# The last token group of a fused RWKV, MLP and soft-MoE kernel worked in two halves, the first one gathered behind step 92

## The reference

```python
# recurrence, per batch and head (4 x 8 x 768 x 48)
cur = einsum('bhd,bhe->bhde', u[None] * kt, vt)
y[:, :, t] = einsum('bhd,bhde->bhe', rt, state + cur)
state = wt[:, :, :, None] * state + einsum('bhd,bhe->bhde', kt, vt)
# dense MLP
h = x @ w_in                                   # 3072x384 @ 384x2048
g = h * clip(h + 3.0, 0.0, 6.0) / 6.0
x2 = g @ w_out
# soft mixture
logits = x2 @ phi                              # 3072 x 32
d = exp(logits - logits.max(0)); d /= d.sum(0) + 1e-09
slot_input = (d.T @ x2).reshape(8, 4, 384)
slot_out[e] = maximum(slot_input[e] @ w1[e], 0.0) @ w2[e]
c = exp(logits - logits.max(1)); c /= c.sum(1) + 1e-09
out = c @ slot_out
```

## Time and profile before

| quantity | us |
| --- | --- |
| median of 3 runs | 408.07 |
| lowest and highest | 407.99, 408.35 |
| the profiled execution | 409.01 |
| its span in the profile | 406.3 |
| TensorE busy in the span | 391.6 |
| VectorE, ScalarE, GpSimd busy | 329.2, 208.1, 210.5 |

### The profile page before, as it was taken

The page is one execution under the profiler, slowest core; times in us unless marked ns, Lnnn a source line. Parts: engine busy times, 40 slices in busy tenths (PEclk is TensorE's granted clock), DMA queues, the critical chain, the costliest instruction groups (busy, mean ns, idle before and its releaser), DMA issues.

```text
span 406.3 us, 10112 instructions
## 1 busy us (share of the span) xinstructions
PE 391.6 (96%) x3977; PEld 210.1 (52%) x3977; DVE 329.2 (81%) x536; ACT 208.1 (51%) x449; POOL 210.5 (52%) x200
## 2 busy tenths in 40 slices
...
GB/s 236 338 407 328 137 67 63 126 235 294 39 128 106 27 124 128 113 20 126 128 115 15 128 114 63 81 128 60 2 2 311 54 423 377 224 298 412 388 112 356
DMA packets 16543, 69.37 MB, mean 171 GB/s; under 512 B 2160, under 2 KB 3184, under 8 KB 14832
## 3 DMA queue, kind: packets, MB, share of 16 engines
...
...
## 4 chain that ended last, share of the span: by engine, by line
PE 74%; DVE 10%; issue 6%; ACT 5%; DMA 2%; POOL 0%; SPq 0%; DVEq 0%; POOLq 0%; ACTq 0%
PE hid L617 13%; PE hid L619 12%; PE hid L618 12%; PE l_ps L665 5%; PE sc_ps L501 4%; PE l_ps L728 3%; PE hid L887 3%; PE inc_ps L530 2%; PE y_ps L600 2%; DVE gated L1076 1%; ACT relu L1495 1%; PE hid L868 1%; PE k_ps L511 1%; PE sc_ps L868 1%; PE y_ps L576 1%
## 5 line engine op out<-in xcount | busy, mean ns | idle before, releaser
L617 PE MATMUL hid<-x_split,w_split 128*128 128x512 f16 x285 | 108.3, 380 | 0.3 <-DVE gated L1076 0.3
L619 PE MATMUL hid<-x_split,w_split 128*128 128x512 f16 x285 | 108.0, 379 | 0.0
L618 PE MATMUL hid<-x_split,w_split 128*128 128x512 f16 x285 | 108.0, 379 | 0.0
L1495 ACT ACTIVATE relu<-hid,three 128x512 f32<-128x512 f32 x95 | 65.1, 685 | 82.2 <-PE hid L619 81.7
L1076 DVE SCALAR_TENSOR_TENSOR gated<-relu,hid 128x512 f32<-128x512 f32 x95 | 64.4, 678 | 24.3 <-ACT relu L1495 23.9
L1097 DVE STREAM_TRANSPOSE ring<-gated 128x512 f32<-128x512 f32 x96 | 68.2, 711 | 3.2
L1701 POOL TENSOR_TENSOR att<-att 128x1024 f16<-128x1024 f32 x20 | 40.2, 2011 | 39.7 <-ACT att L1383 39.7
L617 PEld LDWEIGHTS hid<-x_split,w_split 128*128 128x128 f16 x285 | 27.7, 97 | 36.7 <-issue 6.3
L619 PEld LDWEIGHTS hid<-x_split,w_split 128*128 128x128 f16 x285 | 27.8, 98 | 33.7
L1710 POOL TENSOR_TENSOR att<-att 112x512 f32<-112x512 f32 x21 | 25.5, 1215 | 36.5 <-DVE att L976 26.9
L618 PEld LDWEIGHTS hid<-x_split,w_split 128*128 128x128 f16 x285 | 27.8, 98 | 24.7
...
## 6 DMA issues: line engine op xcount, KB each, us to landing
...
att<-w_dram SPq DMA_DIRECT2D x3, 1536.0 KB, 9.6
...
stage<-w_in_dram SPq DMA_DIRECT2D x2, 1536.0 KB, 13.9
...
```

The source lines that it names most:

```text
L617: pe.matmul(hid[s % 2][:], high, x_high, start=(q == 0), stop=False)
L618: pe.matmul(hid[s % 2][:], high, x_low, start=False, stop=False)
L619: last = pe.matmul(hid[s % 2][:], low, x_high, start=False, stop=(q == KT - 1))
L1495: nc.scalar.activation(relu_tile(s), hid[s % 2][:], ACT.Relu, bias=three[:], scale=GATE / H_SCALE)\
```

## The change

The last group (LAST = 80 = its first step) is worked in two halves of tokens throughout. Steps 80 to 87 make all 16 tiles for the first 256 tokens, two tiles in a step, steps 88 to 95 those for the second. Each step has 18 products of 128 x 256 in place of nine of 128 x 512. The logits are added two steps (four products) at a time, behind the steps listed in `LAST_LOGITS`. The first half's logits are copied, folded, lowered, exponentiated, transposed and summed at steps 89 to 91, and its gather (32 products 32 x 512) stands on TensorE behind step 92 (`gather_half(0, r)`). ScalarE copies the four banks of sums to `dg_half` at steps 93 and 94. Behind step 95 the second half does the same with its own maximum and a second scale `late_alpha`, and its gather of 32 products goes to four other banks (`late_dg_bank`). The fold takes three parts: `acc`, `dg_half` and `dg_last`. The inverse sum is applied later, as the scale of ScalarE's `slot_part` copy.

```diff
+LAST = STEPS - FT
+HALF_STEPS = FT // 2
+GH = GT // 2
-        c_bank = [hid[1], hid[0], sc_bank[1]]
+        late_dg_bank = [y_ps[:, :], inc_ps[:, :], hid[0][:, :], hid[1][:, :]]
+        fold_bank = sc_bank
+        c_bank = [sc_bank[0], hid[0], sc_bank[1]]
+        LAST_LOGITS = {4: 0, 5: 1, 7: 2, 8: 3, 10: 4, 12: 5, 14: 6}
...
+            def half_tile(to, i, half):
+                tokens = (EARLIER, LATER)[half]
+                for q in range(KT):
+                    high, low = w16[:, i, 0, q, :], w16[:, i, 1, q, :]
+                    x_high, x_low = (x16[:, (C - 1) % 2, a, q, tokens] for a in range(2))
+                    pe.matmul(to, high, x_high, start=(q == 0), stop=False, skip_group_check=True)
+                    pe.matmul(to, high, x_low, start=False, stop=False, skip_group_check=True)
+                    last = pe.matmul(to, low, x_high, start=False, stop=(q == KT - 1), skip_group_check=True)
+                return last
...
+                if s >= LAST:
+                    half, pair = divmod(i, HALF_STEPS)
+                    for t in range(2):
+                        last = half_tile(hid[s % 2][:, t * GH:(t + 1) * GH], 2 * pair + t, half)
...
+            def gather_half(half, r):
+                if r == 0:
+                    pe.wait_ge(gated_turned, LAST + HALF_STEPS * (half + 1))
+                    pe.wait_ge(weight_turned, C + half)
+                    pe.wait_ge(acc_added, 4 * (C - 1))
+                    if half:
+                        pe.wait_ge(logits_done, C)
+                        pe.wait_ge(cT_done, 1)
+                for a in range(4):
+                    for c in range(4):
...
+                if s >= LAST and i in LAST_LOGITS:
+                    add_last_logits(LAST_LOGITS[i], range(4))
+                if s == LAST + HALF_STEPS + 1:
                     fold_last_logits(0)
+                if s == STEPS - 4:
+                    for r in range(2):
+                        gather_half(0, r)
...
+            add_last_logits(7, (0, 1))
+            add_last_logits(7, (2, 3))
+            last_natural_logits(0)
+            fold_last_logits(1)
+            last_natural_logits(1)
+            turn_c(1)
+            stay_warm(2, k_ps)
+            for r in range(2):
+                gather_half(1, r)
             for half in range(2):
                 for a in range(4):
                     fold_earlier(a, half)
+                for a in range(4):
+                    fold_first_half(a, half)
                 for a in range(4):
                     fold_last(a, half)
-            stay_warm(1, y_ps)
+            stay_warm(1, k_ps)
             for half in range(2):
                 apply_w_out(half)
-            stay_warm(2, y_ps)
+            turn_c(0, 0, 5)
...
+            half_maximum(1)
+            copy_cT(1)
+            turn_half_weight(1)
+            sum_half_weight(1)
...
+            def weigh_half(half):
+                g, tokens = C - 1 + half, (EARLIER, LATER)[half]
+                act.wait_ge(neg_max_done, g + 1)
+                act.wait_ge(run_sum_done, C - 1)
+                nc.scalar.activation(weight[:, tokens], last_l[half], ACT.Exp, bias=run_neg[g % 2]).then_inc(weight_done, 1)
...
+                if s in (STEPS - 3, STEPS - 2):
+                    first = 2 * (s - STEPS + 3)
+                    for a in range(first, first + 2):
+                        act.wait_ge(dg_ready, 16 * C)
+                        nc.scalar.activation(dg_half[a], dg_bank[a], ACT.Copy).then_inc(dg_half_copied, 1)
```

344 lines of the change are left out of this document (179 added, 165 removed).

## The result

The changed kernel takes **411.97 us** (median, 411.55 to 413.23), the kernel before 408.21 beside it: a ratio of 1.0093, interval 1.0069 to 1.0117. It is slower by 3.8 us; 411.1 was forecast, with 409.7 to 412.6 around it. The sign and the mechanism came out as predicted. But that the stages which the prediction prices add up to +3.1 for +3.0 is in part luck, since its terms missed by 0.7 us in each direction, and another 1.0 us was lost in a place that it did not look at.

The account below looks back on a forecast made before the run. TensorE was taken to bound the steps and the gather onward, with a latency chain between. Terms 4.42 - 0.24 - 2.15 + 1.05 - 0.05 gave +3.0 us on the median of 408.07: 411.1 us, range 409.7 to 412.6.

Parts of the forecast that it names:

- The third rival: Steps 86 to 95 move at the pace of relu and gate, so insertions cost nothing; 407.1 us, chance 0.05.
- The clock, the fourth: Behind step 95 the emptier tail lets TensorE's clock fall, slowing gather and folds; 414 to 416 us, chance 0.05.
- 1, products of 256 columns: In nine steps, 18 products replace nine and add 0.03 us a step; +0.27 us.
- 2, logits: In the steps, five insertions of four products at 0.65 replace two of eight at 1.10; +1.05 us.
- 3, the fold: Between steps 89 and 90, the first half's logits are folded; +0.6 us, bounds 0.5 and 0.75.
- 4, the first gather: Behind step 92, 32 products, half a whole gather, plus switching once more; +2.35 us, bounds 2.2 and 2.6.
- 5, the softmax ahead of the gates: First half's maximum, exponential and sums delay gates 90 and 91, mostly covered by logits; +0.15 us, bounds 0 and 1.2.
- 6, ScalarE's copies: Copies of the first sums behind the relu of steps 93 and 94; no cost, without cover at most 0.5 us.
- 7 and 8, from step 95 to the gather, and the gather: Fewer logit passes but a tile copy before the second gather, -0.24 us; 32 gather products for 64, -2.15 us.
- 9, the folds: Behind the second gather, 24 fold products replace 16 at 0.13 us each; +1.05 us, lower bound 0.
- 10, the projection to the experts: Five transposes replace two unread products, and small softmax instructions just fit beside; -0.05 us, upper bound +0.5.
- 11, loads: The loads of w2 for the experts land early enough that nothing waits for them; 0 us.

Follow-up runs that it names:

- e3: The changed kernel with the first half's gather done twice behind step 92, the second over the first; 413.14 us, ratio 1.0123 to the kernel before.
- e1: The changed kernel with the first half's gather moved from behind step 92 to places behind step 95; 411.38 us, ratio 1.0064 to the kernel before.
- e2: The changed kernel with the last group's logits inserted in eights instead of fours, three insertions fewer; 412.12 us, ratio 1.0103 to the kernel before.

## Why the prediction was right, and where it was not

**The bound** (first part): right. Work in the steps is paid in full (e3: 2.11 for 32 products; e1: 2.28 back). The third rival, slack on TensorE, falls with that. The clock, the fourth, stayed at 1.00 from 353 to 365, with TensorE busy for 3.73 us of the 4.90 behind step 95; the tail did not get as empty as the rival had it. Step 95 starts 4.14 later behind step 86, for 4.42.

**1, products of 256 columns**: steps are 1.97 apart for 1.94; +0.27, right.

**2, logits**: 0.66 for four in all five places, 1.10 for eight: +1.10 against +1.05, right.

**3, the fold**: 2.41 less 1.97 is +0.43; forecast 0.6, under its lower bound of 0.5. The chain's 0.64 holds the time in which the next instruction already overlaps.

**4, the first gather**: 2.35, as forecast.

**5, the softmax ahead of the gates**: 0.00 for 0.15. Gate 90 is 0.9 late, where I had 0.8, and covered: it ends at 342.69, 0.13 ahead of step 92. The changed kernel's rows:

```profile
341.29 0.68 ACT L1554 ACTIVATE relu<-hid,three 128x512 f32<-128x512 f32 x1
...
342.00 0.69 DVE L1124 SCALAR_TENSOR_TENSOR gated<-relu,hid 128x512 f32<-128x512 f32 x1 [1.30 <-ACT relu L1554]
...
344.24 0.68 DVE L1124 SCALAR_TENSOR_TENSOR gated<-relu,hid 128x512 f32<-128x512 f32 x1
```

In the earlier trace rows I had the steps off by one: 340.23 and 342.17 start steps 92 and 93, and the relu and gate are those of step 91. The distances, 1.94 and 0.33, and what follows from them stand. Against the earlier trace rows, the gate waits 1.30 in place of 0.51; gate 91 ends at 344.92, and the logits that need it start at 344.88 with products of another tile. e2 shows what it costs without cover, 0.43 twice.

**6, ScalarE's copies**: nothing, right (e1). They take 0.59 and overlap:

```profile
350.57 0.59 ACT L1687 ACTIVATE ring<-l_ps 128x512 f32<-128x512 f32 x1
351.05 0.60 ACT L1687 ACTIVATE ring<-sc_ps 128x512 f32<-128x512 f32 x1
```

**7 and 8, from step 95 to the gather, and the gather**: -0.20 and -2.11 for -0.24 and -2.15, right.

**9, the folds**: +0.69 for +1.05. The step that failed is the price of 0.13 a product, read from a stretch in which the products in part waited for the copies. A set of four costs 0.43, 0.11 each, and two more sets are 0.87; some of it fills what was waiting before. The folds themselves took 2.78 us, 361.70 to 364.48, between the 3.1 that was to show the step right and the 2.1 to 2.6 that were to show it wrong.

**10, the projection to the experts**: +0.52 for -0.05, just over its upper bound of +0.5, and not for the reason given. The small VectorE instructions did fit. 0.1 is the scale of ScalarE's copies, which I had priced at nothing ("still one instruction"); 0.37 is the late first copy of VectorE, unexplained.

**11, loads**: 0, right.

**"Step 86 keeps its start"**: right, 19.67 us behind step 79's last product for 19.63.

**Not in the sum**: +1.00 in the output, by the place of a code fetch. This is more than the 0.8 us by which the time lies above the forecast. Without it, the stages give +3.1 for the forecast +3.0, and that agreement is partly luck: parts 3, 5 and 9 came out 0.68 below their values, part 10 alone 0.57 above and the small rest another 0.2. Within the range the number so doesn't speak for the single terms; the stages do.
